# Attention and two gated MLPs on one core: a unit's weighing one slot further from its scores, and GpSimd's low parts of the weights in four instructions

## What is computed

```python
scores = scale * np.matmul(q, k.transpose(0, 1, 3, 2))
keep = is_sink | in_window            # 4 sinks, 128 tokens back
a = np.exp(scores - max); a = a / (np.sum(a, axis=-1, keepdims=True) + 1e-09)
attn_out = np.matmul(a, v)
# MLP 1: d_model 512, d_ff 2048
h = x @ w_in;  g = h * (1.0 / (1.0 + np.exp(-1.702 * h)));  x = g @ w_out
# MLP 2: d_model 512, d_ff 1536
gate = 1.0 / (1.0 + np.exp(-(x @ w_gate)));  val = x @ w_val;  out = gate * val @ w_out
```

## Time and profile before

| | |
|---|---|
| time, median of 3 runs | 768.0 us (766.9 to 769.53) |
| time of the profiled execution | 769.46 us |
| its span, from the first to the last instruction | 767.7 us |
| TensorE matmul busy | 704.5 us, 92% of the span |
| VectorE busy | 430.0 us, 56% |
| ScalarE busy | 310.1 us, 40% |
| GpSimd busy | 320.2 us, 42% |
| mean granted TensorE clock | 0.988 |

### The profile page before, as it was taken

The page is one execution under the profiler, slowest core; times in us unless marked ns, Lnnn a source line. Parts: engine busy times, 40 slices in busy tenths (PEclk is TensorE's granted clock), DMA queues, the critical chain, the costliest instruction groups (busy, mean ns, idle before and its releaser), DMA issues.

```text
span 767.7 us, 10351 instructions
## 1 busy us (share of the span) xinstructions
PE 704.5 (92%) x3632; PEld 563.2 (73%) x3632; DVE 430.0 (56%) x1032; ACT 310.1 (40%) x643; POOL 320.2 (42%) x167
## 2 busy tenths in 40 slices
PE   6777999998889988999999899998999999999998
PEld 5566777776667767787777667776778888788886
DVE  6898577777755544367877765645433323431212
ACT  4776434435344424343444444443423232422221
POOL 2563335345435425243543543542324443534330
PEclk9999999999999999999999999999999999999999
DMA  6322332342322322133225242320114324422101
GB/s 204 108 70 84 117 114 68 111 145 102 109 106 80 98 75 96 35 132 123 69 97 165 82 123 97 113 80 29 55 55 137 103 91 145 143 83 83 41 1 55
DMA packets 23795, 73.38 MB, mean 96 GB/s; under 512 B 3616, under 2 KB 3616, under 8 KB 23744
## 3 DMA queue, kind: packets, MB, share of 16 engines
q1 hardware_dynamic: 23744, 72.73, 29.0%
HBM read 69.57 MB, written 3.15 MB: 95 GB/s over the span
## 4 chain that ended last, share of the span: by engine, by line
PE 62%; DVE 21%; issue 8%; ACT 7%; SPq 1%; DMA 0%; ACTq 0%; DVEq 0%
PE ps L746 15%; PE ps L748 15%; PE ps L747 15%; DVE probs_sink L565 6%; DVE pt_lo L550 3%; DVE probs_n L567 3%; PE ps L731 3%; PE ps L812 3%; PE ps L813 3%; PE ps L814 3%; DVE g_hi L591 2%; DVE g_lo L593 2%; ACT probs L427 2%; DVE gated L584 2%; ACT pt_hi L437 1%
## 5 line engine op out<-in xcount | busy, mean ns | idle before, releaser
L372 POOL TENSOR_TENSOR w_lo<-w_raw,w_hi 128x1024 fp32r<-128x1024 f32 (+1 forms) x84 | 241.4, 2874 | 335.3 <-ACT w_hi L421 335.3
L746 PE MATMUL ps<-x_hi,w_hi 128*128 128x512 f32 x480 | 194.8, 406 | 0.7 <-DVE x_lo L577 0.3
L747 PE MATMUL ps<-x_lo,w_hi 128*128 128x512 f32 x480 | 188.7, 393 | 0.0
L748 PE MATMUL ps<-x_hi,w_lo 128*128 128x512 f32 x480 | 188.3, 392 | 0.0
L421 ACT ACTIVATE w_hi<-w_raw 128x1024 fp32r<-128x1024 f32 (+1 forms) x84 | 104.3, 1242 | 173.2 <-PE ps L748 105.1
L584 DVE SCALAR_TENSOR_TENSOR gated<-squashed,ps 128x512 f32<-128x512 f32 x84 | 57.3, 682 | 146.6 <-PE ps L748 84.5
L748 PEld LDWEIGHTS ps<-x_hi,w_lo 128*128 128x128 f32 x480 | 90.6, 189 | 20.1
L746 PEld LDWEIGHTS ps<-x_hi,w_hi 128*128 128x128 f32 x480 | 90.8, 189 | 16.3 <-issue 1.1
L747 PEld LDWEIGHTS ps<-x_lo,w_hi 128*128 128x128 f32 x480 | 91.0, 190 | 14.2
L565 DVE TENSOR_SCALAR probs_sink<-probs,inverse 128x4 f32<-128x4 f32 x96 | 85.8, 893 | 2.6 <-DVE inverse L559 0.3
L427 ACT ACTIVATE probs<-scores,neg_max 128x260 f32<-128x260 f32 x96 | 48.7, 507 | 86.7 <-DVE neg_max L540 86.2
(11 more groups left out here) (73 smaller groups left out, 1035.5 us busy)
## 6 DMA issues: line engine op xcount, KB each, us to landing
w_raw<-in_w SPq DMA_DIRECT2D x36, 768.0 KB, 4.3
w_raw<-in_w SPq DMA_DIRECT2D x48, 512.0 KB, 3.3
q_raw<-in_q_t SPq DMA_DIRECT2D x48, 128.0 KB, 3.7
k_raw<-in_k_t SPq DMA_DIRECT2D x48, 128.0 KB, 3.5
v_raw<-in_v_t SPq DMA_DIRECT2D x12, 256.0 KB, 3.5
out_x<-out_sb SPq DMA_DIRECT2D x12, 256.0 KB, 2.9
v_sink_raw<-in_v_sink SPq DMA_DIRECT2D x2, 160.0 KB, 2.7
k_sink_raw<-in_k_sink SPq DMA_DIRECT2D x4, 8.0 KB, 2.1
```

Of the source, the lines that this page charges most:

```text
L372: pool.tensor_tensor(w_lo[:, slot, 0:n], w_raw[:, slot, 0:n], w_hi[:, slot, 0:n].bitcast(F32), ALU.subtract).then_inc(w_ready, 1)
L746: pe.matmul(ps[:, bank, :], hi, act_hi, start=first, stop=False)
L747: pe.matmul(ps[:, bank, :], hi, act_lo, start=False, stop=False)
L748: return pe.matmul(ps[:, bank, :], lo, act_hi, start=False, stop=last)
```

## The change

Two things. First, the table of offsets: the weighing of unit n - 2 (`W_LAG` = 2) is at quantum 1 of slot n, where it was unit n - 1 at quantum 6; `x_high` and `x_low` are at quantum 2 where they were at 7, and in the lists of ScalarE and VectorE they stand ahead of the pieces at 4. The splits of values (`v_high_part`, `v_low_parts`) and their load are one unit later. A chunk's woven part has one slot more, which holds only a weighing. Second, `weights_low` makes a tile's low part in `W_PARTS` = 4 instructions over a quarter of the columns each, each of which adds 1 to `w_ready`; whoever waits for `w_ready` waits for four times the count.

```diff
--- before.py
+++ after.py
@@ -28,6 +28,7 @@
 RING = 4
 AHEAD = RING - 1
 LOADED = 2 * RING - 1
+W_PARTS = 4
 SINK_ROWS = 80
 MASKED = -1e30
 REGULAR, FIRST = 0, 1
@@ -59,8 +60,9 @@
 
 
 HOLE = 15
-OFF_SCORE, OFF_NORMALISE, OFF_TRANSPOSE, OFF_WEIGH = 0, 2, 3, 6
-OFF_SPLIT, OFF_PT, OFF_X = 1, 4, 7
+OFF_SCORE, OFF_WEIGH, OFF_NORMALISE, OFF_TRANSPOSE = 0, 1, 2, 3
+OFF_SPLIT, OFF_X, OFF_PT = 1, 2, 4
+T_LAG, W_LAG = 1, 2
 
 
 def slot_base(n):
@@ -71,7 +73,7 @@
 
     if c == NCH - 1:
         return []
-    return [(off, n) for n in range(CHUNK_UNITS + 1) for off in range(8) if slot_base(n) + off == q]
+    return [(off, n) for n in range(CHUNK_UNITS + W_LAG) for off in range(8) if slot_base(n) + off == q]
 
 
 class Flow:
@@ -273,7 +275,7 @@
             def load_weights(step):
                 r, slot = step % PER_CHUNK, step % RING
 
-                wait_from(sp, w_ready, step - RING + 1)
+                wait_from(sp, w_ready, W_PARTS * (step - RING + 1))
                 n = columns_of(step)
                 sp.dma_start(w_raw[:, slot, 0:n], w1[r, :, :] if r < F1 else w2[r - F1, :, :]).then_inc(w_loaded[slot], 16)
 
@@ -306,7 +308,7 @@
                             if off == OFF_SPLIT and n < CHUNK_UNITS:
                                 if u % GROUP == 2 and u // GROUP + 2 < 2 * TILES:
                                     load_qk(u // GROUP + 2)
-                                if u % H == 3 and u // H + 1 < TILES:
+                                if u % H == 4 and u // H + 1 < TILES:
                                     load_v(u // H + 1)
                 for tt in range(CH // P):
                     sp.wait_ge(odd_copied if tt % 2 else even_copied, 2 * c + tt // 2 + 1)
@@ -369,8 +371,10 @@
             def weights_low(step):
                 slot, n = step % RING, columns_of(step)
                 pool.wait_ge(w_hi_ready, step + 1)
-                pool.tensor_tensor(w_lo[:, slot, 0:n], w_raw[:, slot, 0:n], w_hi[:, slot, 0:n].bitcast(F32),
-                                   ALU.subtract).then_inc(w_ready, 1)
+                part = n // W_PARTS
+                for at in range(0, n, part):
+                    pool.tensor_tensor(w_lo[:, slot, at:at + part], w_raw[:, slot, at:at + part],
+                                       w_hi[:, slot, at:at + part].bitcast(F32), ALU.subtract).then_inc(w_ready, 1)
 
             for n in range(early.slots):
                 queries_and_keys, values = early.splits(n)
@@ -392,7 +396,7 @@
                             if off == OFF_SPLIT and n < CHUNK_UNITS and u >= CHUNK_UNITS + GROUP and u // GROUP + 1 < 2 * TILES:
                                 if u % GROUP == 0:
                                     qk_low_parts(u // GROUP + 1)
-                                if u % GROUP == 1:
+                                if u % GROUP == 2:
                                     v_low_parts(u // GROUP + 1)
 
         @block.scalar
@@ -494,12 +498,12 @@
                     if off == OFF_SPLIT and n < CHUNK_UNITS and u >= CHUNK_UNITS + GROUP and u // GROUP + 1 < 2 * TILES:
                         if u % GROUP == 0:
                             qk_high_parts(u // GROUP + 1)
-                        if u % GROUP == 1:
+                        if u % GROUP == 2:
                             v_high_part(u // GROUP + 1)
-                    if off == OFF_PT and n > 0:
-                        transposed_high(u - 1)
-                    if off == OFF_X and n > 0 and (u - 1) % GROUP == GROUP - 1:
-                        x_high((u - 1) // GROUP)
+                    if off == OFF_X and n >= W_LAG and (u - W_LAG) % GROUP == GROUP - 1:
+                        x_high((u - W_LAG) // GROUP)
+                    if off == OFF_PT and 0 <= n - T_LAG < CHUNK_UNITS:
+                        transposed_high(u - T_LAG)
 
             for c in range(NCH):
                 for r in range(PER_CHUNK):
@@ -653,12 +657,12 @@
                         normalise(u)
                         if u + 1 == TPS * H:
                             k_sinks(1)
-                    if off == OFF_PT and n > 0:
-                        pt_low(u - 1)
-                    if off == OFF_X and n > 0 and (u - 1) % GROUP == GROUP - 1:
-                        x_low((u - 1) // GROUP)
-                        if u == TPS * H:
+                    if off == OFF_X and n >= W_LAG and (u - W_LAG) % GROUP == GROUP - 1:
+                        x_low((u - W_LAG) // GROUP)
+                        if u - W_LAG + 1 == TPS * H:
                             v_sinks(1)
+                    if off == OFF_PT and 0 <= n - T_LAG < CHUNK_UNITS:
+                        pt_low(u - T_LAG)
 
             for c in range(NCH):
                 for r in range(PER_CHUNK):
@@ -755,7 +759,7 @@
             def hidden(step, k):
                 c, r = divmod(step, PER_CHUNK)
                 if k == 0:
-                    pe.wait_ge(w_ready, step + 1)
+                    pe.wait_ge(w_ready, W_PARTS * (step + 1))
 
                     wait_from(pe, gate_done, step if r == 0 else step - 1)
                     if r == 0:
@@ -822,10 +826,10 @@
                     u = CHUNK_UNITS * (c + 1) + n
                     if off == OFF_SCORE and n < CHUNK_UNITS:
                         score(u)
-                    if off == OFF_TRANSPOSE and n > 0:
-                        transpose(u - 1)
-                    if off == OFF_WEIGH and n > 0:
-                        weigh(u - 1)
+                    if off == OFF_TRANSPOSE and 0 <= n - T_LAG < CHUNK_UNITS:
+                        transpose(u - T_LAG)
+                    if off == OFF_WEIGH and n >= W_LAG:
+                        weigh(u - W_LAG)
 
             pe.wait_ge(idle_ready, 1)
             keep_clock(IDLE_AT_START, IDLE_BANK)
```

## The result

The changed kernel takes 719.33 us in the median (718.94 to 720.15, 4 runs) against 767.52 us (766.9 to 769.53, 4 runs), a ratio of 0.9369 with a 95% interval of 0.9349 to 0.9389. The profiled execution took 719.18 us and its span is 717.4 us.

The account below looks back on a forecast made before the run. TensorE, busy 92%, bounds the kernel with its work and waits, led by the weighing's for pt_lo. Terms of -47.7 plus 2 us gave -45.7, 769.5 to 723.8, median-adjusted 722.3, stated 723; range 714 to 733, all cases 713 to 742.

Parts of the forecast that it names:

- The weighing, -40.7 us: Woven units: 2.3 us more room removes all 52 waits of the weighing's loads for pt_lo, saving 40.7 us.
- The scores, +1 us: Scores of u + 2 now meet pt_lo first; waits beyond 1.4 us return, 2 us, or 1 with shorter holds.
- The masks, -4 us: Woven transposes waiting for the mask: shorter GpSimd holds take away 4 of 5.4 us, bounds 0 and 5.4.
- The clock, -3 us: Stretches at half clock behind the two longest waits disappear with those waits: 3 us gained, bounds 0 and 3.4.
- New short waits, +2 us: TensorE arrives earlier at every other wait while ScalarE and VectorE keep their pace: 2 us allowed.
- The early part, -1 us: Early part, 12.0 us of waits for probs_n: quarters take 1 us away, bounds 0 and 4.
- Quarters: Low parts in four GpSimd instructions let VectorE in between: masks 4 us, early part 1 us, scores 2 lowered to 1.
- rival C: GpSimd's four quarters hold VectorE as one, 0.65 us longer; only the weighing's gain stays: 731 us, chance 0.09.
- GpSimd's extra work: Quarters add 55 us of work on GpSimd, covered by its idle time ahead of them: cost 0 on the path.
- x_high and x_low, cost 0 at 2: The pair, moved from 7, precedes one pt_lo in four, covered by the weighing's room: cost 0, otherwise 13 us.
- B: The wait moves to TensorE's scores or transposes, for pt_lo or the mask; half of 40.7 returns: 743 us, chance 0.12.
- D: Quarters hold off VectorE's four instructions per unit more often, the mask comes later: slower, up to 780 us, chance 0.04.

Follow-up runs that it names:

- with one quantum: The kernel before with the weighing one quantum later (7 instead of 6), nothing else: 738.3 us, ratio 0.9615.
- two quanta and the scores later: The kernel with the new offsets and whole low parts, but the weighing directly behind the next scores: 730.3 us, ratio 0.9506.
- eighths: The changed kernel with each low part in eight instructions instead of four: 723.7 us, ratio 0.9398.
- x behind pt: The changed kernel with x_high and x_low at quantum 5, behind pt_hi and pt_lo, instead of at 2: 729.9 us, ratio 0.9488.

## Why the prediction was right, step by step

**The weighing, -40.7 us: right.** Its wait is gone in full with the offsets alone, and the rest of the span is 40.2 us shorter there. The correction of the printed wait by 0.27 us a time was needed: uncorrected, the loads' row says 54.7, the matmuls' row 30.8, and the starts say 40.9. It also held for a part of the room (25.1 us measured, 25.7 from the list, with one quantum). What had no term is the second matmul of a weighing that waited, 2.6 us. And the room of 2.3 us exists in slots of eight quanta only; it was enough because the waits above 1.6 us all stand in such slots.

**The scores, +1 us: 3.1 in the changed kernel by starts,** and 7.3 where the low parts are whole, against the 2 us put for that case. The step that failed is the distance: "two quanta (1.4 us) behind the old place of the weighing" is one quantum, 0.69 us, in a slot of seven, as worked out under the offsets alone.

**The masks, -4 us: -4.8** (5.4 to 0.6). The quarters were to bring all of it. The offsets alone took 2.6 and left 2.8, the quarters alone took 2.8 and left 2.6.

**The clock, -3 us: the size came out, the reason is not shown.** The stretches of 0.5 at 299 and 436 us are gone, and the granted clock is 1.00 from 88 us to the last microseconds. But they do not stand "behind each of the two longest waits": the second longest is 1.84 us at 187.29 (above), longer than the 1.81 of the earlier trace rows, and the clock behind it is 1.00, as this view of the kernel before shows.

```profile
187.20:190.60 3.40, 3.31 (x20) 2.84 (x21) 2.19 (x6) 1.20 (x1) 0.00 (x0) 1.00 0.56 215
```

The kernel with the quarters only keeps a wait of 2.08 us at 290.70, at a clock of 1.00 from there on. The kernel before itself varies: its executions at a mean clock of 0.993 took 766 to 768 us, those at 0.986 to 0.989 took 768 to 771. So part of the 3 us belongs to the profiled execution, and it is part of why the medians differ by 48.2 and the spans by 50.3.

**New short waits, +2 us:** most of it is `g_lo`, 3.0 us against 0.8 before by the printed rows, 1.7 us more by starts.

**The early part, -1 us: not shown, and 2.7 by the luck of the clock.** The part has one slow stretch of 3.4 us in the changed kernel's profile and three in that of the kernel before. With low parts in one instruction and one such stretch at the same place, 71 us, it ends at 84.0 too (two quanta and the scores later), so there the quarters bring nothing. With three such stretches it ends at 86.7 and 86.4 with whole tiles in the early part and at 85.0 to 86.3 with quarters, but at other places of the stretches; a share of up to 1 us can't be excluded. What sets their number from profile to profile was not settled. This and the woven part's own rest (47.5 us against 44.7 forecast without the 1 us) are the 4.5 us or so by which the two spans differ more than forecast.

**Quarters: the size was about right, the place was not seen.** The prediction had them gain through masks (4), early part (1), scores (1) and, by its rival C, the clock (3), 9 us in all. Measured on top of the offsets are 8.8 us in the medians and 7.3 behind the early part, 4.2 of it at the scores; the slow stretches behind the early part are gone with the offsets alone. GpSimd's extra work is covered, as said, and smaller: 41 us where 55 were worked out. A tile of four took 2.88 us where 3.06 was worked out, since the four overlap a little. TensorE waits for `w_ready` not even with eighths.

**x_high and x_low, cost 0 at 2: it cost nothing, but the reasoning missed a wait.** The text named `pt_lo` as what stands behind `x_low`. What decides, as the kernel with x behind pt shows, is the next group's weighing, which waits for the bank; three quanta later in the list costs 9 us.

**The rivals.** B (the wait moves) exists at 3.1 us, not at 20. C (the four held as one) is refuted: `probs_sink` is let in behind the second quarter and lasts 1.08 us at most, where it was 2.75; the kernels with one and four parts differ. The reading of the Trainium skill's rule (SBUF — State Buffer, "Who interferes with whom") as the order of queues is therefore wrong here, while its hold for a whole instruction agrees: `probs_sink` ends at 353.39, 0.03 us behind the whole `w_lo`. D (slower) found no place: the waits for the mask fell, from 5.4 to 0.6 us.

## What to carry to other kernels

When an engine in order waits for a result, list its waits one by one and sum what a move of one, two or three places would take from each: that gave the time of each of the four moves of the weighing within 4 us here. Take the room of each wait from the list at that very place, since slots of seven and of eight quanta gave 4.6 us of difference at the scores. Cutting a long instruction of one engine into pieces helps the engine that it holds off only where the hold outlasts the slack behind it; first give slack, then see which holds still reach the bottleneck (here cutting those of MLP 2 brought 6.2 of 7.3 us). A piece of work that is moved has two neighbours, the one that waits for its result and the one that waits for its buffer, and the second was the dearer one here.

## What the runs showed that was not expected

The early part's length goes with the number of slow stretches of TensorE's clock in it: 84.0 us with one (granted clock 0.98), 85.5 and 85.6 with two, 85.0 to 86.7 with three, 88.0 with four (0.92), in kernels whose TensorE list for that part is the same. Two profiles of the same changed kernel have one and three (two of the three without a pause), 84.0 and 85.0 us. The difference of 4 us between quarters and eighths lies there, and with one more idle matmul a unit it was gone (clock 1.00, 84.2 us). Why one execution meets more such stretches than another stays open. Splitting each span at a fixed point of the program showed this: behind that point the two profiles of the changed kernel agree to 0.1 us.
